# Six widths instead of four for the experts' first layer, chosen by a tree of branches

## The chip, the cores and the metric

The kernel runs on one core of a Trainium2 chip. The metric is the device time of one execution in microseconds (us); each kernel is run several times, and the median counts.

## What is computed

An attention layer feeds a mixture of experts. Attention has 4 batches, 8 heads, 576 positions and 64 columns a head, a causal window of 128 positions and a bias that falls with the distance. Its output is laid out as 2304 rows of 512 columns. Each row goes to one of 8 experts:

```python
logits = x @ w_gate                          # 2304 x 8
expert_idx = np.argmax(logits, axis=1)
...
h = np.maximum(np.einsum('ecd,edf->ecf', disp, w1), 0.0)   # 512 -> 1024
y = np.einsum('ecf,efd->ecd', h, w2)                       # 1024 -> 512
...
out[i] = gate_w[i] * y[expert_idx[i], pos[i]]
```

An expert takes at most 576 rows. How many rows each gets depends on the data; it is known only while the kernel runs.

## The kernel before

The first part of the kernel is attention with the gate's logits; near its end the rows are ranked by expert. Then TensorE goes through the experts one after the other, in the order 0 to 7. The first tile of 128 rows of expert 0 has code of its own, before the others; behind it `group(n, ...)` is called once for each expert. An expert's rows are gathered from memory by GpSimd into up to three tiles of 128 rows (`gathered`), turned by TensorE (`turn_rows`, line 1478) and split by ScalarE and VectorE into an upper and a lower part (`rowsT_hi`, `rowsT_lo`). The weights are split in the same way, expert n + 1's while expert n is multiplied.

`group` has ten steps. In step c (for c below 8) `first_layer(n, tokens, c)` makes chunk c of the hidden layer: 128 of the 1024 hidden columns, as stationary weights, against `tokens` columns of turned rows. `product` (line 1485) issues three matmuls for each of four slices of the 512 input columns (upper by upper, upper by lower, lower by upper), so twelve a chunk, each with a weight load of its own. ScalarE turns the chunk into its upper part (`relu`, line 857), VectorE makes the lower one (`lower`, line 1182); both always work over all 384 columns. Two steps later the second layer multiplies the chunk, one product of three matmuls, 512 columns wide, for each tile of 128 rows (`second_layer`, `last_chunks`), and adds it up in `y_ps(i)`. In steps 3 to 5 the next expert's tiles are turned. The last expert's last three chunks go tile by tile, so that the first tile is done early.

How wide the first layer is depends on the expert's number of rows. VectorE compares the counts with thresholds and leaves a number for each expert in `third_i` (lines 1153 to 1157):

| rows of the expert | `third` | first layer | second layer |
|---|---|---|---|
| up to 256 | 0 | 256 columns | 2 tiles |
| 257 to 320 | 1 | 320 columns | 3 tiles |
| 321 to 352 | 2 | 352 columns | 3 tiles |
| over 352 | 3 | 384 columns | 3 tiles |

TensorE loads the number (`third_of`) and asks for it by branches in every step (lines 1554 to 1564): one branch for `third > 0` around all the three-tile code, inner ones for its width, and one for `third < 1` around the two-tile code. Where there is no third tile, TensorE adds to the semaphores itself that the third tile's instructions would have added to. Expert 0 is always run at two tiles, with no branch. If an expert has more rows than fit, a loop at the end takes the rest.

Of the kernel before, what the change touches and what calls it, by code (L numbers as in the profile page):

```python
# [23 lines left out]
I32 = mybir.dt.int32  # L24
ALU = mybir.AluOpType
# [9 lines left out]
def attention_moe(nc, q, k, v, w_gate, w1, w2, capacity, out):  # L35
# [14 lines left out]
    SIDE = 3  # L50
    TABLE = -(-N // P)
    RINGED = 3
    TURNED_AT = (3, 4, 5)
    CONSTS = 12
    PAIR = P + 2 * E
# [34 lines left out]
    with ctx:  # L90
        def sb(name, shape, dt=F32):
            return ctx.enter_context(nc.sbuf_tensor(name, shape, dt))
# [70 lines left out]
        src_f = sb("src_f", [P, COLS])  # L163
        src_row = sb("src_row", [P, COLS], I32)
        dst_row = sb("dst_row", [P, COLS], I32)
        third_i = sb("third_i", [P, E], I32)
        taken = sb("taken", [P, 1])
        extra = sb("extra", [P, E])
        extra_to = sb("extra_to", [P, E])
# [198 lines left out]
        def parity(n):  # L368
            return n % 2 if isinstance(n, int) else 0
# [520 lines left out]
        def _(dve):  # L890
# [3 lines left out]
            def link(ins):  # L894

                steps[0] += 1
                ins.then_inc(dve_step, 1)
                dve.wait_ge(dve_step, steps[0])
# [237 lines left out]
            def first_lower(half):  # L1136
# [13 lines left out]
            vec.tensor_scalar(taken[:, :], is_full[:, :], 1.0, None, ALU.subtract)  # L1150
            link(vec.tensor_scalar(tiles_of[:, :], filled[:, :], ROUND_TO_128, 1.0 / P, ALU.subtract, ALU.mult))
            counts = late_ranks_ps[:, E * FULL:E * FULL + E]
            link(vec.tensor_scalar(extra[:, :], counts, float(P * (SIDE - 1)), None, ALU.is_gt))
            link(vec.scalar_tensor_tensor(out=extra[:, :], in0=counts, scalar=float(P * (SIDE - 1) + HALF),
                                          in1=extra[:, :], op0=ALU.is_gt, op1=ALU.add))
            vec.scalar_tensor_tensor(out=third_i[:, :], in0=counts, scalar=float(P * SIDE - HALF // 2),
                                     in1=extra[:, :], op0=ALU.is_gt, op1=ALU.add).then_inc(sizes_ready, 1)
            first_lower(1)

# [116 lines left out]
        def _(pe):  # L1276
# [204 lines left out]
            def product(dst, left, right, first, last):  # L1481


                for n, (a, c) in enumerate(((0, 0), (0, 1), (1, 0))):
                    ins = te.matmul(dst, left[a], right[c], start=first and n == 0, stop=last and n == 2)  # L1485
                return ins

            def weights(slot, kind, at, size):
                return weights_sb[:, slot, kind, at:at + size]

            def first_layer(n, tokens, c):
                for d in range(DC):
                    last = product(hiddenT_ps(c, tokens), [weights(parity(n), kind, F * d + P * c, P) for kind in (0, 1)],
                                   [part[:, d, 0:tokens] for part in rowsT[parity(n)]], d == 0, d == DC - 1)
                last.then_inc(hidden_done, 1)

            def second_layer(n, size, c):
                if c == 0:
                    pe.wait_ge(w_split[1], n * CHUNKS + CHUNKS)
                    if not (isinstance(n, int) and n == 0):  # L1500
                        pe.wait_ge(y_ready, tiles_before(n))
                pe.wait_ge(hiddenT_ready, n * FC + c + 1)
                for i in range(size):
                    last = product(y_ps(i), [part[c % RINGED][:, P * i:P * i + P] for part in hiddenT],
                                   [weights(parity(n), kind, D * c, D) for kind in (2, 3)], c == 0, c == FC - 1)
                    if c == FC - 1:
                        last.then_inc(y_done[i], 1)

            def last_chunks(n, size):

                for i in range(size):
                    for c in range(FC - RINGED, FC):
                        if i == 0:
                            pe.wait_ge(hiddenT_ready, n * FC + c + 1)
                        last = product(y_ps(i), [part[c % RINGED][:, P * i:P * i + P] for part in hiddenT],
                                       [weights(parity(n), kind, D * c, D) for kind in (2, 3)], False, c == FC - 1)
                    last.then_inc(y_done[i], 1)

            def step(n, size, c):

                if c < FC:
                    first_layer(n, P * size, c)
                later_step(n, size, c)

            def later_step(n, size, c):

                by_tiles = isinstance(n, int) and n == E - 1
                if by_tiles and c == FC + RINGED - 2:
                    last_chunks(n, size)
                elif RINGED - 1 <= c < (FC - 1 if by_tiles else FC + RINGED - 1):  # L1530
                    second_layer(n, size, c - (RINGED - 1))

            def rows_and_weights(n):
                pe.wait_ge(rowsT_ready, all_count(n))
                pe.wait_ge(w_split[0], n * CHUNKS + CHUNKS)

            def turn_third(n, third):

                with pe.If(third > 0):
                    turn_rows(n, SIDE - 1)  # L1540
                with pe.If(third < 1):
                    pe.wait_ge(rowsT_ready, tile_count(n, 0))
                    pe.sem_inc(rows_turned[SIDE - 1], 1)

            def third_of(n):
                return pe.value_load(third_i[0:1, n:n + 1], min_val=0, max_val=3)

            def group(n, third):
                after = third_of(n + 1) if n + 1 < E else None
                for c in range(FC + RINGED - 1):  # L1550
                    if third is None:
                        step(n, SIDE - 1, c)
                    else:
                        with pe.If(third > 0):
                            if c < FC:
                                with pe.If(third < 2):
                                    first_layer(n, P * SIDE - HALF, c)
                                with pe.If(third > 1):
                                    with pe.If(third < 3):
                                        first_layer(n, P * SIDE - HALF // 2, c)  # L1560
                                    with pe.If(third > 2):
                                        first_layer(n, P * SIDE, c)
                            later_step(n, SIDE, c)
                        with pe.If(third < 1):
                            step(n, SIDE - 1, c)
                            if c == FC + RINGED - 2:
                                pe.sem_inc(y_done[SIDE - 1], 1)
                    if c in TURNED_AT[:-1] and n + 1 < E:
                        turn_rows(n + 1, c - TURNED_AT[0])
                    if c == TURNED_AT[-1] and n + 1 < E:  # L1570
                        turn_third(n + 1, after)
                return after
# [53 lines left out]
            first_second_layer(range(FC - 2, FC)).then_inc(first_y_done, 1)  # L1626
            rows_and_weights(0)
            pe.wait_ge(sizes_ready, 1)
            third = group(0, None)
            pe.wait_ge(first_y_ready, 1)  # L1630
            for n in range(1, E):
                rows_and_weights(n)
                third = group(n, third)
            pe.wait_ge(tables_ready, 1)
            rest = pe.value_load(rest_i[0:1, 0:1], min_val=0, max_val=TABLE)
            with pe.If(rest > 0):
# [30 lines left out]
```

## Time and profile before

| | |
|---|---|
| time, median of 3 runs | 388.81 us (388.73 to 388.84) |
| the profiled execution's own time | 388.75 us |
| its span, from the first to the last instruction | 387.0 us |
| TensorE busy | 370.0 us, 96% of the span |
| VectorE busy | 252.1 us, 65% |
| ScalarE busy | 202.2 us, 52% |
| GpSimd busy | 145.1 us, 37% |
| memory traffic | 64.90 MB, 168 GB/s over the span |

In the rows PE is TensorE's matmuls, PEld its weight loads, DVE is VectorE, ACT ScalarE, POOL GpSimd, and PEldq is the sequencer that reads TensorE's program. A row such as `128x512 f32 x480 | 118.5, 393` says 480 instructions of 512 columns, busy for 118.5 us together, 393 ns each. Matmuls overlap, so the mean duration of one is not what it adds to the time.

### The profile page before, as it was taken

How to read it: one execution, taken by the hardware profiler on the slowest of the kernel's cores; microseconds unless marked ns; L12 is line 12 of the kernel's file. 1: busy time of each engine (PE TensorE's matmuls, PEld its weight loads, DVE VectorE, ACT ScalarE, POOL GpSimd, SP SyncE). 2: the span in 40 equal slices, each digit the busy share in tenths (PEclk: the TensorE clock that was granted, in tenths of full speed). 3: DMA queues.
4: the chain of work that ended last, by engine and by line, in shares of the span. 5: the costliest groups of instructions: out<-in, count | busy, mean ns of one | idle time of the engine just before them, and what ended most of it. 6: DMA issues, size and time to landing. Idle time of an engine off the chain costs nothing.

```text
span 387.0 us, 8491 instructions
## 1 busy us (share of the span) xinstructions
PE 370.0 (96%) x2978; PEld 318.8 (82%) x2978; DVE 252.1 (65%) x798; ACT 202.2 (52%) x535; POOL 145.1 (37%) x192
## 2 busy tenths in 40 slices
PE   7999999998999998999999999999999999999990
PEld 6787778876877677989989989988989998989980
DVE  6788677799978763767966547556777775542120
ACT  2978878887777612664635424444637644411100
POOL 7558989945643342423042043034033240011011
PEclk9999999999999999999999999999999999999996
DMA  8999999999851111687687365664776666001001
GB/s 163 202 320 204 226 227 232 256 257 218 187 85 56 55 29 56 205 256 257 197 268 229 117 200 179 171 180 169 241 257 232 191 221 209 2 28 45 3 25 51
DMA packets 81326, 64.90 MB, mean 168 GB/s; under 512 B 63982, under 2 KB 63982, under 8 KB 81264
## 3 DMA queue, kind: packets, MB, share of 16 engines
q1 hardware_dynamic: 73600, 52.19, 51.0%
q0 software_dynamic: 3840, 11.03, 8.6%
q10 hardware_dynamic: 3824, 0.80, 1.2%
q8 instruction: 46, 0.75, 0.9%
q14 instruction: 16, 0.13, 0.1%
HBM read 54.56 MB, written 11.02 MB: 169 GB/s over the span
## 4 chain that ended last, share of the span: by engine, by line
PE 78%; POOL 10%; DVE 5%; issue 2%; DMA 2%; ACT 1%; SPq 1%; DVEq 0%; POOLq 0%
PE ps L1485 59%; PE ps L1343 4%; PE ps L1316 4%; POOL weights_sb L617 4%; PE ps L1354 3%; PE ps L1282 2%; PE ps L1478 2%; PE ps L1324 2%; DMA q_rows<-in_q 2%; POOL probsT L624 2%; POOL v_step L605 2%; POOL weights_sb L616 2%; DVE ps L907 1%; DVE probs L920 1%; PE ps L1400 0%
## 5 line engine op out<-in xcount | busy, mean ns | idle before, releaser
L1485 PE MATMUL ps<-weights_sb,hiddenT 128*128 128x512 f32 x480 | 118.5, 393 | 0.0
L1485 PE MATMUL ps<-rowsT_hi,weights_sb 128*128 128x256 f32 (+2 forms) x512 | 115.0, 303 | 1.0 <-DVE rowsT_lo L1163 1.0
L1485 PEld LDWEIGHTS ps<-weights_sb,hiddenT 128*128 128x128 f32 x480 | 87.6, 188 | 16.6 <-DVE hiddenT L1182 0.2
L857 ACT ACTIVATE hiddenT<-ps 128x384 fp32r<-128x384 f32 (+1 forms) x64 | 30.6, 478 | 111.8 <-PE ps L1485 111.6
L1485 PEld LDWEIGHTS ps<-rowsT_hi,weights_sb 128*128 128x128 f32 x512 | 85.8, 188 | 2.6 <-issue 1.4
L1190 DVE TENSOR_TENSOR weights_sb<-raw,weights_sb 128x1024 fp32r<-128x1024 f32 x56 | 68.4, 1222 | 17.1 <-ACT weights_sb L845 16.9
L1485 PE MATMUL ps<-rowsT_lo,weights_sb 128*128 128x256 f32 (+2 forms) x256 | 76.7, 300 | 0.0
L1182 DVE SCALAR_TENSOR_TENSOR hiddenT<-ps,hiddenT 128x384 fp32r<-128x384 f32 (+1 forms) x64 | 34.5, 539 | 56.0 <-ACT hiddenT L857 55.8
L845 ACT ACTIVATE weights_sb<-raw 128x1024 fp32r<-128x1024 f32 x56 | 58.9, 1052 | 0.0
L682 POOL DMA_INDIRECT gathered<-x_rows,src_row x21 | 23.1, 1098 | 91.9 <-DVE weight_now L1176 87.3
L743 ACT ACTIVATE probs<-probs,mins 128x128 f32<-128x128 f32 x144 | 55.6, 392 | 0.6 <-DVE mins L920 0.4
L696 POOL DMA_INDIRECT out<-y_sb,dst_row x21 | 24.0, 1144 | 80.0 <-DVE y_sb L1196 76.4
L1485 PEld LDWEIGHTS ps<-rowsT_lo,weights_sb 128*128 128x128 f32 x256 | 48.1, 188 | 1.2
L624 POOL TENSOR_SCALAR_AFFINE_SELECT probsT<-probsT 128x512 f32<-128x512 f32 x32 | 20.4, 636 | 42.0 <-ACT probsT L769 40.5
L1316 PE MATMUL ps<-kT,qT 64*64 64x192 f32 (+3 forms) x480 | 28.8, 332 | 0.0
L743 ACT ACTIVATION_READ_ACCUMULATOR probs<-probs,mins 128x1 f32 x144 | 27.7, 192 | 0.0
L1354 PE MATMUL ps<-eye_wg,mixT 128*128 128x144 f32 x144 | 24.2, 291 | 2.6 <-DVE mins L920 2.6
L769 ACT ACTIVATE probsT<-ps 128x512 f32<-128x512 f32 x36 | 21.4, 595 | 10.2 <-PE ps L1324 10.2
L907 DVE COPY_PREDICATED ps<-later,ps 128x256 f32<-128x256 int32 (+1 forms) x64 | 22.1, 391 | 5.2 <-PE ps L1316 5.1
L949 DVE TENSOR_TENSOR x_sb<-ps,inv_sums 128x256 f32<-128x256 f32 x36 | 15.3, 424 | 15.5 <-PE ps L1354 13.6
L1196 DVE TENSOR_SCALAR y_sb<-ps,weight_now 128x512 f32<-128x512 f32 x23 | 16.1, 746 | 14.0 <-PE ps L1485 14.0
L1343 PE MATMUL ps<-probsT,v_rows 128*64 128x128 f32 x288 | 23.7, 285 | 0.3 <-issue 0.2
(175 smaller groups left out, 489.0 us busy)
## 6 DMA issues: line engine op xcount, KB each, us to landing
raw<-in_moe_w SPq DMA_DIRECT2D x64, 512.0 KB, 4.7
q_rows<-in_q SPq DMA_DIRECT2D x16, 256.0 KB, 5.9
v_rows<-in_v SPq DMA_DIRECT2D x16, 256.0 KB, 5.4
x_rows<-x_sb SPq DMA_DIRECT2D x16, 256.0 KB, 4.9
k_rows<-in_k SPq DMA_DIRECT2D x14, 256.0 KB, 6.3
k_rows<-in_k ACTq DMA_DIRECT2D x2, 256.0 KB, 7.0
v_rows<-in_v SPq DMA_DIRECT2D x4, 128.0 KB, 5.8
v_front<-in_v SPq DMA_DIRECT2D x4, 128.0 KB, 6.2
```

The lines of the kernel that those rows point to most:

```text
L624: g.affine_select(out=probsT[:, 1, :, :], in_=probsT[:, 0, :, :], compare_op=ALU.is_gt, fill=0.0, base=0, pattern=[[0, QUAD], [-1, P]], ch ...
L696: g.indirect_dma_start(out, bass.IndirectOffsetOnAxis(ap=rows[:, i:i + 1], axis=0), y_sb[:, i, :], None, bounds_check=N - 1, oob_is_err=Fa ...
L743: last = nc.scalar.activation(pr, pr, ACT.Exp, bias=mins[:, kk % 2, n:n + 1], scale=-1.0, accum_out=sums[:, i, h:h + 1])
L845: nc.scalar.activation(weights_sb[:, parity(e), 2 * layer, RAW * j:RAW * (j + 1)], raw[:, j, :], ACT.Copy).then_inc(w_hi[layer], 1)
L857: nc.scalar.activation(hiddenT[0][c % RINGED][:, 0:P * size], hiddenT_ps(c, P * size), ACT.Relu).then_inc(hiddenT_hi, 1)
L907: vec.copy_predicated(both[:, :, 2 * P - earlier[i]:2 * P], later[:, own].bitcast(I32).unsqueeze(1).broadcast_to([P, 2, earlier[i]]), both ...
L1182: vec.scalar_tensor_tensor(out=hiddenT[1][c % RINGED][:, 0:P * size], in0=hiddenT_ps(c, P * size), scalar=0.0, in1=hiddenT[0][c % RINGED][ ...
L1190: vec.tensor_tensor(weights_sb[:, parity(e), 2 * layer + 1, part], raw[:, j, :], weights_sb[:, parity(e), 2 * layer, part].bitcast(F32), A ...
L1316: ins = te.matmul(scores_ps(kk % 2, odd)[rows, 2 * P * n + first:2 * P * n + last], qT[part, u % 2, h // 2, rows], keys, start=True, stop= ...
L1343: last = te.matmul(mixT_ps[DH * odd:DH * odd + DH, n, :], left[:, DH * h:DH * h + DH], probsT[:, part, 2 * odd + n, :], start=(part == 0), ...
L1354: last = te.matmul(back_ps(kk % 2)[:, c, :], mixT[:, c, :], eye_wg[:, 2 * quad + c, :], start=True, stop=True)
L1485: ins = te.matmul(dst, left[a], right[c], start=first and n == 0, stop=last and n == 2)
```

## The change

The table of widths becomes `WIDTHS = (192, 224, 256, 320, 352, 384)`. VectorE compares each count with the first five of them and leaves a kind from 0 to 5 in `kind_i`, with five operations where there were three. Kinds 0 to 2 have two tiles, kinds 3 to 5 (from `WIDE` on) three.

In each step TensorE now asks first whether the kind is below `WIDE`, and then, in `width_of`, once or twice more for the width, as an if with an else. The second layer stands once for all kinds: both tiles that every expert has, and then a branch for the third (`y_tile`, `y_chunks`, `y_begin`). The order of the products within a step stays the same, as do the tiles that are turned and the waits. The second layer multiplies whole tiles of 128 rows in every kind.

```diff
--- before.py
+++ after.py
@@ -50,6 +50,8 @@
     SIDE = 3
     TABLE = -(-N // P)
     RINGED = 3
+    WIDTHS = (192, 224, 256, 320, 352, 384)
+    WIDE = 3
     TURNED_AT = (3, 4, 5)
     CONSTS = 12
     PAIR = P + 2 * E
@@ -163,7 +165,7 @@
         src_f = sb("src_f", [P, COLS])
         src_row = sb("src_row", [P, COLS], I32)
         dst_row = sb("dst_row", [P, COLS], I32)
-        third_i = sb("third_i", [P, E], I32)
+        kind_i = sb("kind_i", [P, E], I32)
         taken = sb("taken", [P, 1])
         extra = sb("extra", [P, E])
         extra_to = sb("extra_to", [P, E])
@@ -1150,10 +1152,11 @@
             vec.tensor_scalar(taken[:, :], is_full[:, :], 1.0, None, ALU.subtract)
             link(vec.tensor_scalar(tiles_of[:, :], filled[:, :], ROUND_TO_128, 1.0 / P, ALU.subtract, ALU.mult))
             counts = late_ranks_ps[:, E * FULL:E * FULL + E]
-            link(vec.tensor_scalar(extra[:, :], counts, float(P * (SIDE - 1)), None, ALU.is_gt))
-            link(vec.scalar_tensor_tensor(out=extra[:, :], in0=counts, scalar=float(P * (SIDE - 1) + HALF),
-                                          in1=extra[:, :], op0=ALU.is_gt, op1=ALU.add))
-            vec.scalar_tensor_tensor(out=third_i[:, :], in0=counts, scalar=float(P * SIDE - HALF // 2),
+            link(vec.tensor_scalar(extra[:, :], counts, float(WIDTHS[0]), None, ALU.is_gt))
+            for width in WIDTHS[1:-2]:
+                link(vec.scalar_tensor_tensor(out=extra[:, :], in0=counts, scalar=float(width),
+                                              in1=extra[:, :], op0=ALU.is_gt, op1=ALU.add))
+            vec.scalar_tensor_tensor(out=kind_i[:, :], in0=counts, scalar=float(WIDTHS[-2]),
                                      in1=extra[:, :], op0=ALU.is_gt, op1=ALU.add).then_inc(sizes_ready, 1)
             first_lower(1)
 
@@ -1494,77 +1497,91 @@
                                    [part[:, d, 0:tokens] for part in rowsT[parity(n)]], d == 0, d == DC - 1)
                 last.then_inc(hidden_done, 1)
 
-            def second_layer(n, size, c):
-                if c == 0:
+            def y_tile(n, i, chunks):
+
+                for c in chunks:
+                    if i == 0:
+                        pe.wait_ge(hiddenT_ready, n * FC + c + 1)
+                    last = product(y_ps(i), [part[c % RINGED][:, P * i:P * i + P] for part in hiddenT],
+                                   [weights(parity(n), kind, D * c, D) for kind in (2, 3)], c == 0, c == FC - 1)
+                if chunks[-1] == FC - 1:
+                    last.then_inc(y_done[i], 1)
+
+            def y_chunks(n, c):
+
+                by_tiles = isinstance(n, int) and n == E - 1
+                if by_tiles and c == FC + RINGED - 2:
+                    return range(FC - RINGED, FC)
+                if RINGED - 1 <= c < (FC - 1 if by_tiles else FC + RINGED - 1):
+                    return range(c - (RINGED - 1), c - (RINGED - 1) + 1)
+                return range(0)
+
+            def y_begin(n, chunks):
+                if chunks[0] == 0:
                     pe.wait_ge(w_split[1], n * CHUNKS + CHUNKS)
                     if not (isinstance(n, int) and n == 0):
                         pe.wait_ge(y_ready, tiles_before(n))
-                pe.wait_ge(hiddenT_ready, n * FC + c + 1)
-                for i in range(size):
-                    last = product(y_ps(i), [part[c % RINGED][:, P * i:P * i + P] for part in hiddenT],
-                                   [weights(parity(n), kind, D * c, D) for kind in (2, 3)], c == 0, c == FC - 1)
-                    if c == FC - 1:
-                        last.then_inc(y_done[i], 1)
-
-            def last_chunks(n, size):
-
-                for i in range(size):
-                    for c in range(FC - RINGED, FC):
-                        if i == 0:
-                            pe.wait_ge(hiddenT_ready, n * FC + c + 1)
-                        last = product(y_ps(i), [part[c % RINGED][:, P * i:P * i + P] for part in hiddenT],
-                                       [weights(parity(n), kind, D * c, D) for kind in (2, 3)], False, c == FC - 1)
-                    last.then_inc(y_done[i], 1)
 
             def step(n, size, c):
 
                 if c < FC:
                     first_layer(n, P * size, c)
-                later_step(n, size, c)
-
-            def later_step(n, size, c):
-
-                by_tiles = isinstance(n, int) and n == E - 1
-                if by_tiles and c == FC + RINGED - 2:
-                    last_chunks(n, size)
-                elif RINGED - 1 <= c < (FC - 1 if by_tiles else FC + RINGED - 1):
-                    second_layer(n, size, c - (RINGED - 1))
+                chunks = y_chunks(n, c)
+                if chunks:
+                    y_begin(n, chunks)
+                    for i in range(size):
+                        y_tile(n, i, chunks)
+
+            def step_of_kind(n, kind, c):
+
+                if c < FC:
+                    with pe.If(kind < WIDE):
+                        width_of(n, kind, c, 0)
+                    with pe.Else():
+                        width_of(n, kind, c, WIDE)
+                chunks = y_chunks(n, c)
+                if chunks:
+                    y_begin(n, chunks)
+                    for i in range(SIDE - 1):
+                        y_tile(n, i, chunks)
+                    with pe.If(kind > WIDE - 1):
+                        y_tile(n, SIDE - 1, chunks)
+                    if chunks[-1] == FC - 1:
+                        with pe.Else():
+                            pe.sem_inc(y_done[SIDE - 1], 1)
+
+            def width_of(n, kind, c, least):
+
+                with pe.If(kind < least + 1):
+                    first_layer(n, WIDTHS[least], c)
+                with pe.Else():
+                    with pe.If(kind < least + 2):
+                        first_layer(n, WIDTHS[least + 1], c)
+                    with pe.Else():
+                        first_layer(n, WIDTHS[least + 2], c)
 
             def rows_and_weights(n):
                 pe.wait_ge(rowsT_ready, all_count(n))
                 pe.wait_ge(w_split[0], n * CHUNKS + CHUNKS)
 
-            def turn_third(n, third):
-
-                with pe.If(third > 0):
+            def turn_third(n, kind):
+
+                with pe.If(kind > WIDE - 1):
                     turn_rows(n, SIDE - 1)
-                with pe.If(third < 1):
+                with pe.Else():
                     pe.wait_ge(rowsT_ready, tile_count(n, 0))
                     pe.sem_inc(rows_turned[SIDE - 1], 1)
 
-            def third_of(n):
-                return pe.value_load(third_i[0:1, n:n + 1], min_val=0, max_val=3)
-
-            def group(n, third):
-                after = third_of(n + 1) if n + 1 < E else None
+            def kind_of(n):
+                return pe.value_load(kind_i[0:1, n:n + 1], min_val=0, max_val=len(WIDTHS) - 1)
+
+            def group(n, kind):
+                after = kind_of(n + 1) if n + 1 < E else None
                 for c in range(FC + RINGED - 1):
-                    if third is None:
+                    if kind is None:
                         step(n, SIDE - 1, c)
                     else:
-                        with pe.If(third > 0):
-                            if c < FC:
-                                with pe.If(third < 2):
-                                    first_layer(n, P * SIDE - HALF, c)
-                                with pe.If(third > 1):
-                                    with pe.If(third < 3):
-                                        first_layer(n, P * SIDE - HALF // 2, c)
-                                    with pe.If(third > 2):
-                                        first_layer(n, P * SIDE, c)
-                            later_step(n, SIDE, c)
-                        with pe.If(third < 1):
-                            step(n, SIDE - 1, c)
-                            if c == FC + RINGED - 2:
-                                pe.sem_inc(y_done[SIDE - 1], 1)
+                        step_of_kind(n, kind, c)
                     if c in TURNED_AT[:-1] and n + 1 < E:
                         turn_rows(n + 1, c - TURNED_AT[0])
                     if c == TURNED_AT[-1] and n + 1 < E:
@@ -1626,11 +1643,11 @@
             first_second_layer(range(FC - 2, FC)).then_inc(first_y_done, 1)
             rows_and_weights(0)
             pe.wait_ge(sizes_ready, 1)
-            third = group(0, None)
+            kind = group(0, None)
             pe.wait_ge(first_y_ready, 1)
             for n in range(1, E):
                 rows_and_weights(n)
-                third = group(n, third)
+                kind = group(n, kind)
             pe.wait_ge(tables_ready, 1)
             rest = pe.value_load(rest_i[0:1, 0:1], min_val=0, max_val=TABLE)
             with pe.If(rest > 0):
```

## Rows read from the trace of the kernel before

**Rows 1.** The page, busy time by engine and in 40 slices.

```profile
PE 370.0 (96%) x2978; PEld 318.8 (82%) x2978; DVE 252.1 (65%) x798; ACT 202.2 (52%) x535; POOL 145.1 (37%) x192
...
PEclk9999999999999999999999999999999999999996
```

**Rows 2.** Chain of waits, 244 to 301 us: start, duration, what.

```profile
249.90 24.09 PE ps L1485 x141
...
277.63 19.71 PE ps L1485 x126
```

**Rows 3.** One window; columns in its first row.

```profile
core 0: us, PE busy (x) PEld busy (x) DVE busy (x) ACT busy (x) POOL busy (x), PEclk, DMA share, GB/s
...
275.00:300.00 25.00, 25.00 (x165) 22.65 (x164) 18.99 (x26) 14.03 (x22) 6.28 (x6) 1.00 0.75 244
```

**Rows 4.** TensorE's matmuls by form, whole span.

```profile
L1485 PE MATMUL ps<-rowsT_hi,weights_sb 128*128 128x256 f32 x256 | 50.3, 285 | 1.0 <-DVE rowsT_lo L1163 1.0
...
L1485 PE MATMUL ps<-rowsT_lo,weights_sb 128*128 128x256 f32 x128 | 35.9, 281 | 0.0
```

**Rows 5.** Timeline of TensorE, expert 4, one step of 256 columns: start, duration.

```profile
280.27 0.28 PE L1485 MATMUL ps<-rowsT_hi,weights_sb 128*128 128x256 f32 x1
...
281.69 1.55 PE L1485 MATMUL ps<-weights_sb,hiddenT 128*128 128x512 f32 x6
283.08 0.28 PE L1485 MATMUL ps<-rowsT_hi,weights_sb 128*128 128x256 f32 x1
```

**Rows 6.** Timeline of TensorE, steps of 320 and of 352 columns.

```profile
241.14 0.31 PE L1485 MATMUL ps<-rowsT_hi,weights_sb 128*128 128x320 f32 x1
...
242.91 2.25 PE L1485 MATMUL ps<-weights_sb,hiddenT 128*128 128x512 f32 x9
...
337.57 0.33 PE L1485 MATMUL ps<-rowsT_hi,weights_sb 128*128 128x352 f32 x1
...
339.50 2.71 PE L1485 MATMUL ps<-weights_sb,hiddenT 128*128 128x512 f32 x11
```

**Rows 7.** Weight loads by form, and fourteen 16-bit ones in the timeline.

```profile
L1485 PEld LDWEIGHTS ps<-rowsT_hi,weights_sb 128*128 128x128 f32 x512 | 85.8, 188 | 2.6 <-issue 1.4
...
L1316 PEld LDWEIGHTS ps<-kT,qT 64*64 64x64 f32 x448 | 14.5, 132 | 4.1
...
L1436 PEld LDWEIGHTS ps<-in_column,in_tile 128*128 128x128 f16 x9 | 0.4, 96 | 0.0
...
139.13 0.42 PEld L1360 LDWEIGHTS ps<-onehot,ones_b 128*128 128x128 bf16 x14 [0.27 <-issue]
```

**Rows 8.** Timeline of the weight loads where the experts' products begin.

```profile
153.34 0.19 PEld L1485 LDWEIGHTS ps<-rowsT_hi,weights_sb 128*128 128x128 f32 x1 [1.44 <-issue]
153.44 0.19 PEld L1485 LDWEIGHTS ps<-rowsT_lo,weights_sb 128*128 128x128 f32 x1
```

**Rows 9.** Full four-byte products of 144 columns: the form, and four in the chain.

```profile
L1354 PE MATMUL ps<-eye_wg,mixT 128*128 128x144 f32 x144 | 24.2, 291 | 2.6 <-DVE mins L920 2.6
...
98.47 0.49 PE ps L1354 x4
```

**Rows 10.** Questions of TensorE's program, by line: min/median/max ns.

```profile
L1554 PEldq COMPARE_BRANCH  x70: 72/73/1099, 174.4 to 369.0; - x70
...
L1564 PEldq COMPARE_BRANCH  x70: 72/211/435, 174.7 to 373.4; - x70
```

**Rows 11.** Waits from 153 to 378 us: total us, times, longest.

```profile
ACT hiddenT L857 <- PE ps L1485: 111.6, 56, 6.7
...
PEld ps L1485 <- issue: 1.4, 1, 1.4
...
PEld ps L1485 <- DVE hiddenT L1182: 0.2, 1, 0.2
```

**Rows 12.** Timeline of VectorE around the last of its thresholds.

```profile
145.99 0.17 DVE L1156 SCALAR_TENSOR_TENSOR third_i<-ps,extra 128x8 int32<-128x8 f32 x1
...
147.67 0.69 DVE L1139 TENSOR_TENSOR first_hiddenT_lo<-ps,first_hiddenT_hi 128x512 fp32r<-128x512 f32 x1 [1.52 <-ACT first_hiddenT_hi L828]
```

## Prediction

> **What bounds the kernel now.** I read the page's busy times first, then the chain of waits, then the stretch of the eight experts by windows, and last the start-to-start times of single instructions. TensorE is busy for 96% of the span at the full clock, the 2.4 GHz level [rows 1]. From the start of the experts' products, 153 us, to their end at 378 us the chain that ended last is nothing but TensorE: pieces such as 126 matmuls in 19.71 us, one after the other [rows 2]. A window inside this stretch has TensorE busy for all of its 25.00 us, while VectorE has 18.99 us of work in it [rows 3]. So in this stretch the time is the number of matmuls times their spacing, and what is taken from a matmul there comes off the span, as long as nobody else becomes late.
>
> The reader should not take the mean duration of a matmul (285 ns at 256 columns [rows 4]) for its price. They are pipelined; the price is the distance between starts. Twelve first-layer matmuls of 256 columns run from 280.27 to 281.69 us, 1.42 us, so 118.3 ns each, and the six second-layer ones behind them, 512 columns wide, from 281.69 to 283.08, so 232 ns each [rows 5]. At 352 columns twelve take 337.57 to 339.50, 160.8 ns each; at 320 columns 241.14 to 242.91, 147.5 ns each [rows 6]. The three widths lie on one line of about 0.45 ns a column: (160.8 - 118.3) / 96 = 0.443 and (147.5 - 118.3) / 64 = 0.456.
>
> **Which experts the change touches.** I worked out the routing from the reference with its first seed: the experts get 373, 244, 350, 293, 183, 193, 328 and 340 rows. The trace agrees: 256 + 128 first-layer matmuls have 256 columns, which is four experts of 96 each (expert 0, always run at two tiles behind its separate first tile, and experts 1, 4, 5) [rows 4]. After the change expert 4 (183 rows) goes to 192 columns, expert 5 (193 rows) to 224. Expert 1 (244 rows) stays at 256, and the wide ones keep 320 and 352, since those thresholds are the old ones. So 96 matmuls go from 256 to 192 columns and 96 from 256 to 224. Nothing else gets narrower: the second layer still multiplies whole tiles of 128 rows, and ScalarE and VectorE still turn over all 384 columns of each chunk.
>
> **What a narrower matmul is worth.** If the spacing went on falling along the line, 192 columns would take 118.3 - 64 x 0.443 = 89.9 ns and 224 columns 104.1 ns: 96 x 28.4 ns = 2.73 us and 96 x 14.2 ns = 1.36 us, together 4.1 us. But every one of these matmuls has a weight load of its own, 128 columns of four-byte values, and the load for the next one starts when the present one starts. No row shows a four-byte load of this width spaced closer than 118 ns in a stream, so its least spacing has to be bounded. From above it is 118.3 ns, what the stream at 256 columns shows. From below I have two readings. First, where TensorE starts empty at 153.34 us, the second load starts at 153.44, when the first matmul gets its weights, 0.10 to 0.11 us later [rows 8]. Second, loads by shape: 188 ns at 128 columns, 132 ns at 64 columns, both four-byte, so 56 ns for 64 columns more, and 112 ns for all 128; with 16-bit weights a load takes 96 ns and fourteen of them go in 0.42 us, (0.42 - 0.096) / 13 = 25 ns each [rows 7]. So the pipeline can space matmuls far closer than 118 ns, and it is the width of the four-byte weights that costs some 0.8 ns a column. A floor between 104 and 118 ns it is; I take 110, by the middle of the two readings.
>
> The Trainium skill (TensorE: Matmul & The Clock Gate, section LDWEIGHTS) states that a load takes its columns divided by 1.2 GHz, an estimate of 106.7 ns here; by it the change would save 192 x 11.6 ns = 2.2 us instead of what I take. That rule speaks against the change as well: below 256 columns there would be little left to win. The rows agree with it within their rounding.
>
> At 110 ns the first layer of both experts costs the same: 192 x (118.3 - 110) = 1.6 us saved. At a floor of 104 ns it would be 192 x 14.2 = 2.7 us, at 118.3 nothing. Notice that 224 columns then lose nothing against 192.
>
> **The branches (questions) in TensorE's program.** Before, a step of a two-tile expert asks two questions (line 1554, answered by a jump over the wide code, and line 1564); a three-tile step asks up to six. After, every step asks whether the kind is below 3, then one or two more in the tree, jumps over the other widths, and asks once for the third tile. A question costs 73 ns when passed and about 211 when it jumps, with a worst of 1099 ns [rows 10]. For experts 4 and 5 that is at most three more, 3 x 0.21 = 0.65 us a step, if it lay bare. It is covered by the queue: in the whole stretch TensorE's weight loads wait for issue once, for 1.4 us at its very start, and the 1099 ns jump left no gap [rows 11]. The cover is work already handed over; a step has 12 x 110 + 6 x 232 = 2.7 us of it. Without cover, 20 steps would cost 13 us. I count nothing. The code per step grows: six widths of 24 instructions (a load and a matmul for each of 12) and 18 for the three tiles of the second layer, 162 against 3 x 24 + 24 + 18 + 12 = 126.
>
> **The thresholds on VectorE.** Two more linked operations of 0.17 us, each 0.2 us from the last, make the chain to the kinds 0.4 us longer. It ends at 146.16 now, and the next operation on that queue, the lower half of the first tile, starts at 147.67 after 1.52 us of idling for ScalarE [rows 12]. So 1.1 us of idling is left; with that gone it would be 0.4 us on TensorE's path. Nothing.
>
> **Who could be late next.** In the narrow experts a step gets 0.1 us shorter (12 x 8.3 ns). ScalarE waits for TensorE 56 times in this stretch, 111.6 us in all, 2.0 us each, and TensorE's side waited for the hidden chunks once, 0.2 us [rows 11]. VectorE's 18.99 of 25.00 us becomes 18.99 of about 24.3. The weights' transfers run at 244 GB/s in that window [rows 3] and need 3% more. Nothing gets in the way. The matmuls to the right of these experts just start earlier, and the last store moves with them.
>
> **Sum.** The profiled execution took 388.75 us: 387.0 us of span and 1.75 us around it, which stay. 387.0 - 1.6 = 385.4, and 385.4 + 1.75 = 387.15, so 387.2 us. The median of the runs shown, 388.81, is 0.06 above this execution, which changes nothing. A difference of less than 0.2%, 0.8 us, can't be told from none here.
>
> **The rivals.**
>
> *No floor.* The spacing follows the line down to 192 columns: -4.1 us, 384.7 us. For it: three widths lie on the line. Against: the two readings of the load. 5%.
>
> *The floor is already reached.* The 118.3 ns at 256 columns is the load's own spacing; then nothing changes, 388.8 us. For it: no load of this kind is seen closer. Against: 118.3 lies on the line of the wider ones, where the matmul decides, and the load on an empty engine took 0.10 to 0.11. Between 110 and 118, the verdict turns at 114.2 ns (0.8 / 192 = 4.2 ns saved). 11%.
>
> *Narrow products lose the one-pass rate.* This is the one that ends slower. The experts' products are of the reduced four-byte type, and no row shows that type under 256 columns. The four-byte products in full precision run at 0.49 us for four of 144 columns, 122.5 ns each, 0.85 ns a column, and each of the 72 products in the code is recorded as two [rows 9]. If the narrow ones fell to 0.85 ns a column, 192 would take 163 ns and 224 190 ns: 96 x 45 + 96 x 72 = 11.2 us more, 400.0 us; with two passes each, 326 and 381 ns, some 45 us more, 434 us. It decides from 118.3 ns on, that is for any rate above 0.62 ns a column. For it: the slope of the wide ones says nothing of a change of mode. Against: nothing in the rows has such a step either. 18%.
>
> *Questions come through.* The Trainium skill (Runtime: NRT & Kernel Launch, section Instruction fetch mechanics) has it that a taken branch to code that isn't fetched yet stalls the sequencer; it would cost here what the worst question shows, in each of the seven experts with a tree. By the rows: the longest question is 1.1 us [rows 10]; one in each of the seven experts, uncovered, gives 7.7 - 1.6 = 6.1 us more, 394.9 us; one or two alone end near the old time. More code lies between the targets than before, which speaks for it; the cover of 2.7 us against it. 6%.
>
> **How the numbers follow.** The floor near 110 has 60%: three parts of it in a hundred end within 0.2%, the rest faster. Faster: 57 + 5 (no floor) = 62%. Same: 3 + 11 (floor reached) + 1 (questions) = 15%. Slower: 18 + 5 = 23%. The range goes from 384.7 (no floor) to 389.6 (the floor reached, with up to two questions bare and the gain lost); it holds 60 + 5 + 11 and most of the questions' case, some 80%. The slow rate lies outside it. The likeliest case alone has 386.0 to 388.8.
>
> **What the trace of the changed kernel would show.** Right: the 96 products of expert 4 at 192 and the 96 of expert 5 at 224 columns in equal spacing near 110 ns, twelve in about 1.32 us; the two experts shorter by 0.8 us each, all the others as before; no new wait for issue or for the hidden chunks. Wrong: a spacing of 90 and 104 (no floor), 118 (floor reached), or 160 and more (slow rate); or gaps ahead of the first matmul of a width, with long questions beside them.

## The result and the profile after

The changed kernel takes 392.38 us (median of 4 runs, 391.44 to 393.26), the kernel before 388.77: a ratio of 1.0089, with a 95% interval of 1.0076 to 1.0102. It is 3.6 us slower where 1.6 us faster was forecast, and outside the range. The profiled execution took 391.44 us with a span of 389.6, so 2.6 us of span are to be accounted for; the other runs were slower still, so the profile shows the least of the loss. One execution of one experiment below (five widths, shift of 126) took 2022 us; nothing on record explains it, and it is left out of every ratio.

The page of the changed kernel, busy time by engine, the granted clock and the queue that fetches programs:

```profile
PE 369.5 (95%) x2978; PEld 317.6 (81%) x2978; DVE 253.0 (65%) x800; ACT 201.8 (52%) x535; POOL 145.5 (37%) x192
...
PEclk9999999999999999999999999999999999999996
...
q8 instruction: 54, 0.88, 0.9%
```

The products' spacing did fall. Two steps of the timeline, expert 4 at 192 columns and expert 5 at 224 (start, duration):

```profile
272.14 0.25 PE L1488 MATMUL ps<-rowsT_hi,weights_sb 128*128 128x192 f32 x1
...
273.46 0.88 PE L1488 MATMUL ps<-weights_sb,hiddenT 128*128 128x512 f32 x3
...
308.88 0.27 PE L1488 MATMUL ps<-rowsT_hi,weights_sb 128*128 128x224 f32 x1
...
310.21 1.09 PE L1488 MATMUL ps<-weights_sb,hiddenT 128*128 128x512 f32 x4
```

Twelve products take 273.46 - 272.14 = 1.32 us at 192 columns, 110 ns each, and 310.21 - 308.88 = 1.33 us at 224, 111 ns each, where 256 columns took 118.3 [rows 5]. Over 192 products that is (8.3 + 7.3) x 96 ns = 1.5 us saved, as forecast. So 2.6 + 1.5 = 4.1 us were lost somewhere.

The chain of waits in the same stretch of time where before there was TensorE alone [rows 2]:

```profile
259.86 8.86 PE ps L1488 x51
268.72 0.60 issue
...
278.64 14.95 PE ps L1488 x102
293.59 1.62 issue
...
318.36 0.42 issue
```

"issue" is time in which TensorE waited for nothing that the profile names: no data, no semaphore. I read it so: the next instructions were not there yet. The waits from 153 to 385 us (total us, times, longest), which answer to [rows 11]:

```profile
PEld ps L1488 <- issue: 5.2, 6, 1.8
...
PE ps L1488 <- issue: 2.6, 3, 1.6
...
PEld ps L1488 <- DVE hiddenT L1185: 0.2, 1, 0.2
```

A weight load waits for issue six times, where it was once; for the hidden chunks it waits as little as before. And the branches, by line (min/median/max ns), which answer to [rows 10]:

```profile
L1555 PEldq COMPARE_BRANCH  x72: 65/208/2441, 174.6 to 368.9; - x72
...
L1558 PEldq COMPARE_BRANCH  x72: 65/176/3602, 174.9 to 370.6; - x72
...
L1538 PEldq COMPARE_BRANCH  x56: 65/211/1950, 174.5 to 368.5; - x56
```

The typical branch still costs 0.2 us, but the longest ones now last 2.4, 3.6 and 2.0 us. The largest gap, in the timeline of TensorE, is read so: a product starts at 293.32 us and the next one only at 295.21:

```profile
293.32 0.28 PE L1488 MATMUL ps<-rowsT_hi,weights_sb 128*128 128x224 f32 x1
295.21 1.17 PE L1488 MATMUL ps<-weights_sb,hiddenT 128*128 128x512 f32 x4 [1.62 <-issue]
```

Start to start that is 1.89 us in place of 0.11: 1.78 us lost. Counted over two spacings, because the first product behind a gap is also followed late, 0.84 us are lost from 268.44 to 269.50 us and 0.68 from 318.04 to 319.04. Another 0.5 us, in expert 1, shows in the chain only as a later start: the same piece of 18 matmuls begins at 189.57 us, where before it began at 189.08. Together 3.8 of the 4.1 us.

Counted from the program's listing, TensorE's program has 12688 instructions after and 10605 before. The page says 54 packets of program against 46, and 0.88 MB / 54 = 16 KB each. 2083 more instructions over 8 more packets are 260 a packet; I take 256, at 64 bytes each. The Trainium skill (Runtime: NRT & Kernel Launch, section Instruction fetch mechanics) gives the same block, 16 KiB or 256 instructions, and says that code is fetched ahead in order. The packets here, 54 of 16 KB, agree with the size; on the order see the version that asks once for each expert.

### The profile page after: what moved, and what is told of

It is laid out like the page before. It is cut to its first block, busy times and chain, and to the rows that moved or that the text cites. A ratio compares the mean times of both kernels' runs of the same rounds, so it can differ in the third digit from the quotient of the medians.

```text
span 389.6 us, 8504 instructions
## 1 busy us (share of the span) xinstructions
PE 369.5 (95%) x2978; PEld 317.6 (81%) x2978; DVE 253.0 (65%) x800; ACT 201.8 (52%) x535; POOL 145.5 (37%) x192
## 4 chain that ended last, share of the span: by engine, by line
PE 76%; POOL 10%; DVE 5%; issue 3%; DMA 2%; SPq 1%; ACT 1%; DVEq 0%; POOLq 0%
PE ps L1488 58%; PE ps L1346 4%; POOL weights_sb L619 4%; PE ps L1319 4%; PE ps L1357 3%; PE ps L1285 2%; PE ps L1481 2%; POOL probsT L626 2%; POOL v_step L607 2%; PE ps L1327 2%; DMA v_rows<-in_v 2%; POOL weights_sb L618 2%; DVE ps L909 1%; SPq L388 1%; DVE probs L922 1%
## 5 line engine op out<-in xcount | busy, mean ns | idle before, releaser
L1488 PE MATMUL ps<-rowsT_hi,weights_sb 128*128 128x352 f32 (+4 forms) x512 | 114.0, 301 | 2.1 <-DVE rowsT_lo L1166 1.0
L1488 PE MATMUL ps<-rowsT_lo,weights_sb 128*128 128x352 f32 (+4 forms) x256 | 76.3, 298 | 0.0
```

## The experiments

The theory: TensorE's program is fetched block by block while it runs. The more unused code lies in each step, the faster the sequencer passes the blocks, and at some of them it gets to a jump before the next block has landed. When the queue of products runs dry meanwhile, TensorE stands. Rivals: the form and number of the branches, the narrow products themselves, and that a fetch takes that long whatever else goes on. "Before" in the ratios is the kernel before, run on the same chip.

**The same code without narrow products.** The copies for 192 and 224 rows multiply 256 columns:

```diff
+                widths = [max(w, 2 * P) for w in WIDTHS]
                 with pe.If(kind < least + 1):
-                    first_layer(n, WIDTHS[least], c)
+                    first_layer(n, widths[least], c)
```

> The changed kernel with every branch, kind and copy of code kept, but the copies for 192 and 224 rows multiply 256 columns. Code theory (TensorE's program, 12688 instructions against 10605 before, has to be fetched across longer jumps, and long branches leave TensorE empty): the stalls stay and only the narrow spacing is lost, 392.4 + 192 x 7 ns = about 393.7 us. Rival, the narrow products cause the loss themselves (they use up the queued work faster, or run slow): about 388.8 us.

Measured: 392.87 us, ratio 1.0079 (1.0056 to 1.0103). The loss is there without any narrow product; that rival is out. The 1.3 us by which it should have been worse than the changed kernel don't show; the two intervals overlap, and these runs spread from 391.79 to 394.13.

**Dead code in the kernel before.**

```diff
                             later_step(n, SIDE, c)
+                            if c < FC:
+                                with pe.If(third > 3):
+                                    first_layer(n, P * SIDE, c)
+                                    for d in range(2):
+                                        product(...)
```

> The kernel before with 36 instructions a step more that are never run, inside the three-tile branch and behind one more branch: 12692 instructions, as many as the changed kernel has. All widths as before. Code theory: 388.8 + about 4.9 (the loss of 3.6 and the 1.3 that narrow products give back) = about 393 us, with long branches in two-tile experts above all. Rivals (the tree with its number of branches; the narrow products): 388.8 to 389.2 us.

Measured: 390.54 us, ratio 1.0038 (1.0013 to 1.0063); 54 packets of program. The 36 instructions a step stand behind a branch that no expert passes. Code that never runs makes the kernel slower, by 1.5 us. Its longest branch on the first line rose to 2957 ns:

```profile
L1554 PEldq COMPARE_BRANCH  x70: 72/73/2957, 174.5 to 371.0; - x70
```

This is under half of the 4.2 us that I expected: the amount of code alone doesn't set the size.

**The tree with the old widths**, `WIDTHS = (256, 320, 352, 384)`, 9776 instructions:

> The changed kernel with the widths of before (256, 320, 352, 384): the tree and the common second layer alone, 9776 instructions, fewer than before. Code theory: 388.8 us or a little less, no branch over 1.1 us left bare. Rival, the form of the tree (if with else, a branch between second and third tile in every step): above 390 us.

Measured: 389.0 us, ratio 0.9986 (0.9965 to 1.0006), 43 packets. The tree for the wide experts and the common second layer cost nothing that can be told (the interval ends 0.2 us above before). In the two-tile experts, where most of the loss lies, a step asks one question less here than in the changed kernel, so for them the form is tested only by the number of branches, below.

**Without the width of 192**, `WIDTHS = (224, 256, 320, 352, 384)`:

> The changed kernel without the width of 192: both narrow experts run at 224 columns, 11232 instructions. Both widths space their products at 111 to 112 ns, so 192 should give nothing over 224. Code theory: 388.8 - 1.3 + a part of the loss, 387.5 to 389.5 us. Rival, the tree's form or the narrow products: 391 us or more.

Measured: 389.58 us, ratio 0.9998 (0.9977 to 1.002). Two bare waits were left in its profile, at the starts of experts 2 and 6, some 1.6 us together, about what the narrow products give.

**Less traffic beside the fetch.** In both kernels the weight transfers of experts 1 to 7 move an eighth of their bytes; these experts then multiply what was left in the buffers, at the same shapes:

```diff
+                if not (isinstance(e, int) and e == 0):
+                    src, dst = (src[:, 0:F // 8], dst[:, 0:F // 8]) if layer == 0 else (...)
                 sp.dma_start(dst, src).then_inc(raw_landed[j], 16)
```

> The kernel before with the weight transfers of experts 1 to 7 cut to an eighth of their bytes (the rest of each buffer keeps what was there, so these experts multiply wrong weights at the same shapes). TensorE sets the experts' stage in every theory, so about 388.8 us, or up to 1 us less; no branch over 0.5 us outside the last one.

> The changed kernel with the same cut. Theory that the fetch of program blocks is late because it shares the transfer engines with the weights: the branches of 1.2 to 3.6 us fall under 0.8 us, the gaps close, and this runs 1.3 us under the light version of before. Rival, the fetch itself takes 3 us and more whatever else is moved, or long jumps cost this anyway: the long branches stay and this runs about 3.5 us over it.

Measured: 388.61 us for the kernel before (ratio 0.9987, 0.9975 to 0.9999) and 387.94 for the changed one (0.9959, 0.9944 to 0.9975). With the same code and the same branches the changed kernel no longer loses 3.6 us but comes out 0.7 us under the other one. Its waits for issue and its longest branches on the three lines of the tree:

```profile
PEld ps L1490 <- issue: 1.9, 2, 1.4
```

```profile
L1557 PEldq COMPARE_BRANCH  x72: 65/208/1441, 175.0 to 365.7; - x72
...
L1560 PEldq COMPARE_BRANCH  x72: 65/176/1008, 175.2 to 367.5; - x72
...
L1540 PEldq COMPARE_BRANCH  x56: 65/211/2223, 174.8 to 365.3; - x56
```

3602 ns became 1008 on the inner line. So the loss needs the traffic beside the fetch. It isn't all: on the outer line, at the start of expert 6, 2.2 us remain where there were 2.0, others of 1.3 to 1.6 us remain too, all over the 0.8 I had expected, and of the 1.5 us that the narrow products give, 0.7 show.

The packets of the program's own queue, in the traces of the two versions of the changed kernel, tell how much of a late fetch is its own time. A packet is in transfer for 0.97 us (median) in both. From its end to the end of the late branch it is 1.3 to 1.5 us in both (branches over 0.65 us: eleven, and nine). What differs is the time from the end of such a branch to the start of the next packet: 0.8 to 2.6 us, median 1.3, with all the weights, and 0.7 to 1.3 us, median 0.75, with an eighth. By these figures I estimate 0.7 + 1.0 + 1.4 = 3.1 us of a fetch as its own and some 0.6 us more, at times near 2, as waiting for its turn beside the weights. Both of the ideas that were tested against each other hold a part. Where the weights hold a packet up before its transfer, whether in the transfer engines or ahead of them, isn't shown.

**More branches, no code behind them.** Three branches a step that all jump:

```diff
+                        for q in range(3):
+                            with pe.If(third > 3 + q):
+                                pe.sem_inc(passed, 0 + 1)
                         with pe.If(third > 0):
```

> The kernel before with three more branches in every step of experts 1 to 7 and next to no code behind them (11025 instructions against 10605): each jumps, 0.63 us a step more in the sequencer. Code theory: the queued products cover it, 388.8 to 389.5 us. Rival, the number of branches empties the queue: 0.2 us and more in most of the 70 steps, over 395 us.

Measured: 389.24 us, ratio 1.0006 (0.9996 to 1.0017). 210 branches more, 0.2 us each by their rows, cost at most 0.7 us by the interval, where 42 us lay in them: the queued products cover short branches nearly whole, as the prediction had it. Not quite: the profile has four short waits for issue more than before, 1.0 us in all, and one branch of 1.9 us:

```profile
PEld ps L1485 <- issue: 2.4, 5, 1.4
```

Whether they come from the branches or from the 420 instructions more that this version has, this run can't say.

**The width asked once for each expert.** All ten steps stand behind it in one piece, five times over:

```diff
+                def pick(widths, least):
+                    ...
+                    with pe.If(kind < least + half):
+                        pick(widths[:half], least)
+                    with pe.Else():
+                        pick(widths[half:], least + half)
```

> Widths 224, 256, 320, 352, 384; the width is asked once for each expert, and all ten steps of the expert stand behind it in one piece, five times over (14684 instructions, of which each expert runs one piece). Code theory, with fetching ahead only in order: no long branch inside an expert, but one to three far jumps at its start, each 2 to 4 us against 2.6 us of queued work: 390 to 400 us. Rival, the total of the code decides: 14684 instructions are 2000 more than the changed kernel has, so above 396 us with stalls inside the experts. If far jumps cost no more than 0.3 us: 387.5 us.

Measured: 427.76 us, ratio 1.096 (1.0922 to 1.0998). Far worse than I expected: 390 to 400 us for the theory. The waits, the branches, and what TensorE does between experts 1 and 2:

```profile
PEld ps L1488 <- issue: 32.0, 8, 8.3
```

```profile
L1606 PEldq COMPARE_BRANCH  x22: 65/83/5262, 174.6 to 411.5; - x22
```

```profile
199.75 1.07 PE L1488 MATMUL ps<-weights_sb,hiddenT 128*128 128x512 f32 x4
208.30 0.65 PE L1488 MATMUL ps<-rowsT_hi,weights_sb 128*128 128x352 f32 x1 [7.48 <-issue]
208.75 0.50 PE L1488 MATMUL ps<-rowsT_lo,weights_sb 128*128 128x352 f32 x1
209.04 0.79 PE L1488 MATMUL ps<-rowsT_hi,weights_sb 128*128 128x352 f32 x2
```

Nine jumps to an expert's piece took 3.7 to 5.3 us, two in a row where an expert needs two, and behind this gap TensorE ran at the lower clock for the next 3 us. Only 46 packets were fetched, for 14684 instructions, which would be 57 of 256 each: pieces that are jumped over whole are not loaded. The stalls stand at the starts of the experts, next to none inside them. This fits fetching ahead in order.

**Moving the blocks.** Instructions that never run ahead of expert 1 shift where each block of 256 begins:

```diff
             kind = group(0, None)
+            with pe.If(kind > 14):
+                for q in range(21):
+                    product(...)
```

> The changed kernel with 126 instructions that are never run put ahead of expert 1's steps, half a block of 256. One branch a block is long in every trace; this moves where in the experts the blocks begin. If where a block begins within a step matters much, the time moves by more than 1 us from 392.4, either way, and the long branches stand elsewhere. Rival, only the amount of code counts: 392 to 393 us.

> Widths 224, 256, 320, 352, 384 with 66 never-run instructions ahead of expert 1. The version without them had two bare waits, 1.5 and 0.5 us, at the starts of experts 2 and 6. If these hang on where the block begins they go, and the narrow spacing shows: 388.8 - 1.3 = 387.5 to 388.3 us. Rival: 389 to 390 us as without the shift.

> The same with 126 never-run instructions. As for 66: between 387.5 and 390 us, and apart from the other shift by more than 0.5 us if the place of the block counts.

Measured: the changed kernel with 126 of them 395.48 us, ratio 1.0162 (1.0141 to 1.0184), 2.8 us over the changed kernel's own 1.0089 by the ratios. The five widths, 0.9998 without a shift, run at 387.66 us with 66 (0.997, 0.9959 to 0.9981) and at 387.81 with 126 (0.9968, 0.9957 to 0.998): faster than before. These are three kernels with the same work for TensorE; apart from one branch that always jumps, only the place of the blocks differs. For the changed kernel the effect is clear of the noise; for the five widths the intervals with and without a shift just touch (0.9977 and 0.9981). I had expected the two shifts to differ by more than 0.5 us, and they differ by 0.15. The chain of the one with 66, in the stretch shown above:

```profile
277.03 19.04 PE ps L1488 x126
...
296.51 1.33 PE ps L1488 x12
297.84 0.10 issue
297.94 1.66 PE ps L1488 x6
...
303.21 16.84 PE ps L1488 x98
```

The piece of 126 matmuls that took 19.71 us [rows 2] takes 19.04, 0.67 us less over seven steps of twelve products, 8 ns each, and 0.10 us is left bare. The same 126 instructions hurt one program and, as far as the noise lets one say, help the other, so there is no good shift in general.

**The copy for 224 columns in every second step only**, 10504 instructions:

> Widths 224, 256, 320, 352, 384, but the copy of the code for 224 columns stands in every second step only: 10504 instructions, about as many as before the change (10605), and half of the narrow spacing, 96 x 6.5 ns = 0.6 us. Code theory: 388.0 to 388.5 us, faster than before. Rival, the tree costs something of its own: 389 us or more.

Measured: 388.74 us, ratio 0.9996 (0.9986 to 1.0007). No gain, against my expectation. With as little code as before it still had one branch of 2.9 us, at the start of expert 6, and 0.6 us bare for issue, just the size of the gain.

**The experts' stage alone.** The whole time also holds the part ahead of the experts, and their first product starts at 152.9 to 154.4 us in the profiles of all these kernels. From that start to the start of the last product the profiles have, one execution of each:

| kernel | instructions, without the shift | stage, us |
|---|---|---|
| before | 10605 | 224.01 |
| before, light traffic | 10605 | 224.05 |
| tree with the old widths | 9776 | 224.05 |
| 224 in every second step | 10504 | 224.29 |
| before, more branches | 11025 | 224.81 |
| before, dead code | 12692 | 225.63 |
| five widths; shift 66; shift 126 | 11232 | 224.54; 223.09; 223.53 |
| changed; shift 126 | 12688 | 226.59; 231.02 |
| changed, light traffic | 12688 | 223.12 |
| changed, no narrow products | 12688 | 229.12 |

The three kernels without a bare wait inside the stage agree within 0.04 us. The order is roughly that of the ratios, and the shifts of the five widths stand apart more clearly than there. The 2.5 us between the last row and the changed kernel are more than narrow spacing gives, but they are the slowest execution of the one and the fastest of the other.

## Why the prediction was wrong

*The floor* was right: 110 ns taken, 110 and 111 ns measured, the same for 192 and 224 columns. No floor, the floor already reached and the slow rate are all ruled out by the spacing.

*The questions in TensorE's program* is the step that failed: "I count nothing". It rested on two things. One was that 2.7 us of queued products cover a branch; the worst branch lasted 3.6 us, and 1.8 us of it were bare, so that only 1.8 were covered there. The 2.7 us hold for a step with a second layer. But an expert opens with 36 first-layer products in a row, three steps' worth, and there a step holds 1.33 us; three of the four losses lie in or at the end of such an opening (behind products 24, 36 and 24 of experts 4, 5 and 6). The other was the price: 1.1 us, the longest branch on two lines of before, was taken for the worst there is. The same profile has one that jumps over the whole loop at the end, with no weights in transfer:

```profile
L1636 PEldq COMPARE_BRANCH  x1: 3323/3323/3323, 374.6 to 374.6; - x1
```

That was the price of a jump to code that isn't there, and it stood under the last products, where it cost nothing. The branch of 1.1 us was the sign of a limit nearby, a block that came late once while the cover was still enough. I had worked out 162 instructions a step against 126 and didn't ask what they mean for the fetch: in a two-tile expert, where a step is shortest, the sequencer reaches a new block soonest, and most of the long branches are there (six of the eleven over 1 us in experts 4 and 5). An estimate from the counts above: in an opening TensorE's 1.33 us a step go with six copies of 24 instructions, so a block of 256 lasts 2.4 us, and before, with four copies and 1.42 us, 3.8 us; the closest packets of the changed kernel's trace start 3.2 us apart. No run tests this by itself, and it doesn't explain the late branch of the version with 224 in every second step, which stands in a wide expert.

*The rival "questions come through"* had the mechanism and the sign. It had 6%, and its price, 1.1 us in each of seven experts, was put together wrongly: the waits are fewer and longer. Expert 3 and the last expert, which loads no weights beside it, have none in the profile.

*Thresholds on VectorE, who could be late next, the sum's other terms* held: the experts' products start at 153.35 us, within 0.01 of before, and no wait for data is new.

What the runs showed in place of the step: narrow products give about 1.5 us; code that isn't run costs 1.5 us in the kernel before (dead code), and in the changed kernel 3.1 us (0.0079 x 388.8, the run without narrow products) to 5.0 us (3.5 by its ratio and the 1.5 given back). What remains open is how the loss divides between the amount of code and its place. The run without narrow products and the dead-code version have nearly the same number of instructions (12688 and 12692) and no narrow product, and lose 3.1 and 1.5 us; the shifts move the time by 1.1 to 2.8 us, so place alone could explain it, but I didn't shift the dead-code version.

The best version found is the five widths with a shift: 0.3% under the kernel before. It hangs on the place of the blocks and on the routing of this data, and an edit elsewhere in TensorE's program may undo it.

## What to carry to other kernels

Code that isn't run has a price when the engine with the long program is also the one that sets the time: count instructions a microsecond, and look at the longest branches of every line rather than at the median one: in the changed kernel each one over 1 us ended 1.3 to 1.5 us behind the end of a packet of program, a block that came late. Before adding a copy of code for a size, ask whether the size gives anything over its neighbour; here 192 gave nothing over 224, the spacing being the same, which fits a floor set by the weight load that both have. And after a change of a long program measure it at two or three shifts, or the place of its blocks is measured with it.

## What the runs showed of the hardware

- Four-byte products of the reduced type at 192 and 224 columns start every 110 to 111 ns, with 128 columns of weights for each: the same for both, against 118.3 ns at 256 columns.
- The program comes in packets of 16 KB, about 256 instructions. In the changed kernel a packet was in transfer for 0.97 us (median); the late branch ended 1.3 to 1.5 us behind it; the next packet started 0.8 to 2.6 us behind that with the weights in transfer, 0.7 to 1.3 us with an eighth of them.
- A branch whose code came late took up to 3.6 us in the changed kernel, 4.3 us with the shift, 2.2 us with an eighth of the weights, 3.7 to 5.3 us when it went over whole pieces, and 3.3 us over the loop at the end of the kernel before, with no weights in transfer.
- After the wait of 7.48 us in the version that asks once for each expert TensorE ran at the lower of its two clocks. Two windows of that kernel (busy times of TensorE, its weight loads, VectorE, ScalarE, GpSimd, then the granted clock, the share of the transfer engines, GB/s):

```profile
208.50:211.50 3.00, 2.80 (x9) 2.34 (x9) 0.00 (x0) 0.00 (x0) 0.00 (x0) 0.50 0.03 5
212.50:216.00 3.50, 3.50 (x24) 3.50 (x23) 2.25 (x3) 2.79 (x4) 0.00 (x0) 1.00 0.02 5
```

At the clock of 0.50, the 1.2 GHz level, the products of 352 columns stood about 290 ns apart by their starts (208.75, 209.04), against 160.8 at the full one.
